# Router logits in column groups: four 384-column fp32 matmuls a chunk in place of twelve 8-column ones

## What is computed

```python
def _moe2_ref(x, modality_id, w_gate, modality_bias, w1, w2) -> np.ndarray:
    N, D = x.shape
    E = w_gate.shape[1]
    logits = x @ w_gate + modality_bias[modality_id]
    e_idx = np.argmax(logits, axis=1)
    ...
    for e in range(E):
        mask = e_idx == e
        ...
        h = np.maximum(x[mask] @ w1[e], 0.0)
        out[mask] = gate_w[mask, None] * (h @ w2[e])
```

## Time and profile before

| | |
|---|---|
| median of 3 runs | 871.68 us |
| the profiled execution's own time | 872.59 us |
| its span, first to last instruction | 870.8 us |
| TensorE (PE) busy | 857.4 us, 98% |
| VectorE (DVE) busy | 519.3 us, 60% |
| ScalarE (ACT) busy | 374.4 us, 43% |
| GpSimd (POOL) busy | 327.0 us, 38% |
| mean granted TensorE clock | 0.997 of full |

### The profile page before, as it was taken

One profiled execution on the slowest core, in us unless ns is written; L12 is line 12 of the kernel. 1 busy time (PEld: TensorE's weight loads), 2 busy tenths in 40 slices (PEclk: granted clock), 3 DMA queues, 4 the chain that ended last, 5 costly groups with the idle time before them and its releaser, 6 DMA issues.

```text
span 870.8 us, 15612 instructions
## 1 busy us (share of the span) xinstructions
PE 857.4 (98%) x5233; PEld 735.9 (84%) x5242; DVE 519.3 (60%) x1401; ACT 374.4 (43%) x945; POOL 327.0 (38%) x372
## 2 busy tenths in 40 slices
PE   8999999999999999999999999999999999999997
PEld 5677898888888888899999999988888888888885
DVE  6975555333453335449787773873877456666664
ACT  6966413545454455543221132143355335554442
POOL 3836762344333443346335332160043221222212
PEclk9999999999999999999999999999999999999999
DMA  8983212222223210242131121537265635565541
GB/s 192 286 205 97 61 48 65 74 65 78 52 52 110 62 38 26 73 157 66 45 97 61 60 74 37 193 98 254 97 195 208 248 135 187 183 223 182 186 133 45
DMA packets 77517, 103.40 MB, mean 119 GB/s; under 512 B 38973, under 2 KB 43069, under 8 KB 77312
## 3 DMA queue, kind: packets, MB, share of 16 engines
q1 hardware_dynamic: 73760, 91.16, 34.2%
q0 software_dynamic: 3680, 11.28, 3.8%
HBM read 92.98 MB, written 10.22 MB: 119 GB/s over the span
## 4 chain that ended last, share of the span: by engine, by line
PE 89%; DVE 5%; DMA 1%; issue 1%; POOL 1%; ACT 1%; SPq 1%; DVEq 0%; ACTq 0%; POOLq 0%
PE ps L1243 32%; PE ps L1282 16%; PE ps L1805 13%; PE ps L1790 12%; PE ps L1174 3%; PE ps L1203 2%; PE ps L1184 2%; PE ps L1815 2%; PE ps L1150 2%; DMA out_raw<-in_moe_w_out 1%; PE ps L1319 1%; PE ps L660 1%; DVE sm L1520 1%; DVE w_lo L2048 1%; PE ps L1312 1%
## 5 line engine op out<-in xcount | busy, mean ns | idle before, releaser
L1035 POOL TENSOR_TENSOR sm<-sm,rinv 72x288 f32<-72x288 f32 (+1 forms) x51 | 45.5, 893 | 175.3 <-DVE rinv L1531 175.2
L1067 POOL TENSOR_TENSOR out_lo<-out_raw,out_hi 128x512 fp32r<-128x512 f32 x72 | 100.6, 1397 | 5.8
L1589 DVE SCALAR_TENSOR_TENSOR h<-h,ps 128x384 f32<-128x384 f32 x72 | 39.8, 553 | 105.2 <-ACT h L1437 104.5
L1065 POOL CAST out_hi<-out_raw 128x512 fp32r<-128x512 f32 x72 | 50.1, 696 | 136.4 <-DMA out_raw<-in_moe_w_out 136.4
L1243 PE MATMUL ps<-x_hi,val_hi 128*128 128x384 f32 x288 | 101.0, 351 | 0.0
L1243 PE MATMUL ps<-x_hi,gate_hi 128*128 128x384 f32 x288 | 100.3, 348 | 0.0
L1243 PE MATMUL ps<-x_hi,gate_lo 128*128 128x384 f32 x288 | 96.9, 336 | 0.0
L1243 PE MATMUL ps<-x_hi,val_lo 128*128 128x384 f32 x288 | 96.5, 335 | 0.0
L1441 ACT ACTIVATE h_hi<-h 128x384 fp32r<-128x384 f32 x72 | 37.8, 525 | 136.5 <-DVE h L1595 136.5
L1243 PE MATMUL ps<-x_lo,val_hi 128*128 128x384 f32 x288 | 96.4, 335 | 0.0
L1243 PE MATMUL ps<-x_lo,gate_hi 128*128 128x384 f32 x288 | 93.8, 336 | 0.0
(11 more groups left out here) (278 smaller groups left out, 1944.5 us busy)
## 6 DMA issues: line engine op xcount, KB each, us to landing
w_raw<-in_moe_w SPq DMA_DIRECT2D x72, 512.0 KB, 4.8
out_raw<-in_moe_w_out SPq DMA_DIRECT2D x72, 256.0 KB, 2.7
x_rows<-y_tiles SPq DMA_DIRECT2D x18, 256.0 KB, 2.7
early_w_raw<-in_moe_w SPq DMA_DIRECT2D x8, 512.0 KB, 8.0
gate_raw<-in_moe_w_gate SPq DMA_DIRECT2D x4, 768.0 KB, 8.1
val_raw<-in_moe_w_val SPq DMA_DIRECT2D x4, 768.0 KB, 10.9
qk<-in_q SPq DMA_DIRECT2D x8, 288.0 KB
qk<-in_k SPq DMA_DIRECT2D x8, 288.0 KB
```

The lines of the kernel that those rows point to most:

```text
L1035: pool.tensor_tensor(s3, s3, rinv[0:n, i, :].unsqueeze(2).to_broadcast([n, 4, c]), ALU.mult).then_inc(s_no, 1)
L1065: pool.tensor_copy(oh[i][:, :], o_raw[i][:, :]).then_inc(s_oh, 1)
L1067: pool.tensor_tensor(ol[i][:, :], o_raw[i][:, :], oh[i][:, :].bitcast(f32), ALU.subtract).then_inc(s_ol, 1)
L1589: dve.scalar_tensor_tensor(out=hf[n % 2][:, :], in0=hf[n % 2][:, :], scalar=1.0, in1=ps[:, 0, 0:CH], op0=ALU.add, op1=ALU.mult).then_inc(s ...
```

## The change

For each of the last three chunks, the roles of the operands are swapped. `rw`, padded with zeros from 8 to 32 columns for each of the four parts of the 512 features, becomes the stationary operand, and `yT` of all three tiles (384 tokens) the moving one. The four parts `kk` of the features are not summed in PSUM: part `kk` is written to the output partitions 32kk to 32kk+31 of one bank. ScalarE copies this to `parts`, three transposes turn it back so that tokens are on partitions, and VectorE sums the four parts with one reduce and adds the bias of three tiles at once.

```diff
-Y_TILE = {(NC - 2, t): at(NC - 1, 1 + t, 0) for t in range(TT)}
-LOGITS = {k: s + 2 for k, s in Y_TILE.items()}
+Y_TILE = {(c, t): at(c + 1, 1, 1) + 2 * t for c in (NC - 3, NC - 2) for t in range(TT)}
+LOGITS = {c: Y_TILE[c, TT - 1] + 3 for c in (NC - 3, NC - 2)}
+TURN_BACK = {c: s + 2 for c, s in LOGITS.items()}
...
-for c in range(NC - 3, NC - 2):
-    free = [at(c + 1, f, 1, 1) for f in range(1, FT) if at(c + 1, f, 1, 1) not in QK_AT]
-    for t in range(TT):
-        Y_TILE[c, t], LOGITS[c, t] = free[t], free[t + 1]
...
-        rw = keep.put("rw", [P, KT, E])
+        rw = keep.put("rw", [P, KT, P // KT])
...
+            pool.memset(rw[:, :, E:P // KT], 0.0).then_inc(s_cst, 1)
...
             def turn_y(c, t):
...
+                if n >= 1:
+                    pe.wait_ge(s_yte, n)
                 for kk in range(KT):
-                    mm = pe.transpose(ps[:, y_bank(c), kk * P:(kk + 1) * P], ys[:, t, kk * P:(kk + 1) * P],
-                                      ident[:, :])
+                    mm = pe.transpose(ps[:, 6, kk * P:(kk + 1) * P], ys[:, t, kk * P:(kk + 1) * P], ident[:, :])
...
-                pe.wait_ge(s_yte, turned(c, t) + 1)
+                pe.wait_ge(s_yte, TT * i + TT)
                 for kk in range(KT):
-                    mm = pe.matmul(ps[:, logits_bank(c), 0:E], yT[:, kk, :], rw[:, kk, :],
-                                   start=(kk == 0), stop=(kk == KT - 1))
+                    mm = pe.matmul(ps[32 * kk:32 * kk + 32, 5, 0:CH], rw[:, kk, :], yT[:, kk, :], start=True, stop=True)
                 mm.then_inc(s_lg, 1)
+
+            def turn_back(c):
+                i = ROUTED.index(c)
+                pe.wait_ge(s_lc, i + 1)
+                for t in range(TT):
+                    mm = pe.transpose(ps[:, 5, t * P:(t + 1) * P], parts[:, t * P:(t + 1) * P], ident[:, :])
+                mm.then_inc(s_lt, 1)
...
+            def copy_parts(c):
+                i = ROUTED.index(c)
+                act.wait_ge(s_lg, i + 1)
+                act.activation(parts[:, :], ps[:, 5, 0:CH], ACT.Copy).then_inc(s_lc, 1)
...
+            def add_bias(c):
+                i, n = ROUTED.index(c), TT * c
+                dve.wait_ge(s_lt, i + 1)
+                dve.tensor_reduce(summed[:, :, :],
+                                  ps[:, 5, 0:CH].rearrange("p (t k e) -> p t e k", t=TT, k=KT)[:, :, 0:E, :],
+                                  axis=AX, op=ALU.add).then_inc(s_ls, 1)
+                dve.wait_ge(s_ls, i + 1)
+                dve.tensor_tensor(logit[:, n:n + TT, :], summed[:, :, :], bias_t[:, n:n + TT, :],
                                   ALU.add).then_inc(s_le, 1)
...
-            last_logits(0)
-            last_logits(1)
+            pe.wait_ge(s_ca, 2)
+            pe.wait_ge(s_cv, 1)
+            for kk in range(KT):
+                mm = pe.matmul(ps[32 * kk:32 * kk + 32, 5, 0:CH], rw[:, kk, :], yT_c[:, kk, :], start=True, stop=True)
+            mm.then_inc(s_cl, 1)
             up(0, range(KT // 2 + 1, KT))
-            last_logits(2)
+            pe.wait_ge(s_cc, 1)
+            for t in range(TT):
+                mm = pe.transpose(ps[:, 6, t * P:(t + 1) * P], parts_c[:, t * P:(t + 1) * P], ident[:, :])
+            mm.then_inc(s_cb, 1)
             turn_h(0)
             up(1, [0])
             pe.wait_ge(s_hot, 2)
...
+            act.wait_ge(s_cl, 1)
+            act.activation(parts_c[:, :], ps[:, 5, 0:CH], ACT.Copy).then_inc(s_cc, 1)
             relu(0)
...
+            dve.wait_ge(s_cb, 1)
+            link(dve, dve.tensor_reduce(summed_c[:, :, :],
+                                        ps[:, 6, 0:CH].rearrange("p (t k e) -> p t e k", t=TT, k=KT)[:, :, 0:E, :],
+                                        axis=AX, op=ALU.add))
+            link(dve, dve.tensor_tensor(logit[:, NTT - TT:NTT, :], summed_c[:, :, :], bias_t[:, NTT - TT:NTT, :],
+                                        ALU.add))
             one_hot(dve, NTT - TT, NTT)
```

More of the change, by code:

```diff
@@ L124 @@
          [("p", j) for j in TURN_AT.get(s, [])] + [("o", j) for j in PV_AT.get(s, []) if s >= EARLY]
[L125 to L126 removed]
+         + [("ss", c) for c in SS_AT.get(s, []) if c] + [("rb", c) for c in SPREAD_AT.get(s, []) if c]]
 BEFORE7 = {x: BANK7[n - 1] if n else None for n, x in enumerate(BANK7)}
[L131 to L134 removed]
 Y_AT = by_tick((k, Y_TILE[k]) for k in sorted(Y_TILE))
[L136 to L138 removed]
+LOGITS_AT = by_tick((c, s) for c, s in LOGITS.items())
+TURN_BACK_AT = by_tick((c, s) for c, s in TURN_BACK.items())
+ROUTED = (NC - 3, NC - 2)
 DOTTED = TT * (NC - 3)
@@ L275, in fused_kernel @@
         kT = [res.put(f"kT{i}", [P, WIN + S]) for i in range(2)]
-        sm = [res.put(f"sm{i}", [P, 512]) for i in range(SM - 1)] + [alias("sm_early", yT_at, [P, 512])]
+        sm = [res.put(f"sm{i}", [P, 512]) for i in range(SM - 1)] + [sm_early]
         pt = [res.put(f"pt{i}", [P, 4 * LQ]) for i in range(2)]
@@ L352, in fused_kernel @@
         dots = ra.put("dots", [P, 2, E])
+        yT = ra.put("yT", [P, KT, CH])
+        parts = ra.put("logit_parts", [P, CH])
+        summed = ra.put("logits_summed", [P, TT, E])
         re = Region(xT_at)
@@ L369, in fused_kernel @@
         rc = Region(vh_at + QB, oh_at)
-        yT_c = [rc.put(f"yT_c{i}", [P, KT, P]) for i in range(TT)]
+        yT_c = rc.put("yT_c", [P, KT, CH])
+        parts_c = rc.put("logit_parts_c", [P, CH])
+        summed_c = rc.put("logits_summed_c", [P, TT, E])
         rank8 = rc.put("rank8", [P, NTT, E])
@@ L1104, in bank_7_free @@
                     pe.wait_ge(s_nv, before[1] + 1)
-                elif before[0] == "rb":
+                else:
                     pe.wait_ge(s_rc, before[1])
[L1107 to L1110, removed]
             def residues():
@@ L1353, in front_pe @@
                     spread_roots(c)
-                for key in LOGITS_AT.get(s, []):
-                    logits(*key)
                 for key in Y_AT.get(s, []):
                     turn_y(*key)
+                for c in LOGITS_AT.get(s, []):
+                    logits(c)
+                for c in TURN_BACK_AT.get(s, []):
+                    turn_back(c)
                 if s == COUNT_1:
@@ L1473, in front_act @@
                     evac_yT(*key)
+                for c in LOGITS_AT.get(s, []):
+                    copy_parts(c)
                 if s == SPREAD[0] + 1:
@@ L1663, in front_dve @@
                     add_bias_to_dots(i)
-                for key in LOGITS_AT.get(s, []):
-                    add_bias(*key)
+                for c in TURN_BACK_AT.get(s, []):
+                    add_bias(c)
                 for val, i in SPLIT_AT.get(s - 2, []):
```

86 lines of the change are left out of this document (31 added, 55 removed).

## The result

The changed kernel takes 868.48 us (median of 7 runs, 867.06 to 872.4), the kernel before, run beside it, 871.95 us (871.12 to 873.11). The ratio is 0.9957, with a 95% interval of 0.9944 to 0.997: 0.43% faster, where 0.35% and 868.7 us were forecast. The same kernel timed twice more gave 868.4 us for 871.85 (ratio 0.9949, 0.9931 to 0.9967) and 868.67 for 871.83 (0.9953, 0.9936 to 0.9969).

A forecast was written before the change was run, and what follows sets the result against it. TensorE, busy 857.4 of 870.8 us, was taken to bound the kernel. Terms -1.20 - 1.32 - 0.77 + 0.27 = -3.0 us take the median from 871.68 to 868.7 us; range 867.9 to 871.2.

The forecast's parts named there:

- chunk 3: TensorE, routing of chunk 3: turning, logits block and turning back take 2.70 us for 3.90, that is -1.20.
- chunk 4: TensorE, routing of chunk 4: turning, logits block and turning back take 2.70 us for 4.02, that is -1.32.
- chunk 5's logits: TensorE, chunk 5: block of 1.02 us replaces two tiles' logits of 1.79, -0.77; turning back free in the relu wait.
- the reduce, paid in full: VectorE's chain to `hot_b`, start of experts' part: added reduce costs +0.27 us (0.21 to 0.33), since TensorE already waits.
- All four groups at once: Logits block on TensorE: four column groups overlap fully, two steps, 0.64 us of streams; chance 0.68 with no new wait.
- serial rival: Logits block: passes run one after another, block 2.95 us, sum +2.8 us, 874.5 us; chance 0.08.
- two-at-once rival: Logits block: only two groups run at once, block 1.66 us, sum -1.1 us, 870.6 us; chance 0.12.
- The fixed price: Logits block on TensorE: going to narrow column groups and back costs 0.37 us, the same for both lengths read.
- What costs nothing: ScalarE's copies, new waits of the turns, GpSimd's memset, SyncE: covered by other work, slack 1 us and more, 0 us.
- new-wait rival: Routing chunks: late `h_lo` or an uncovered copy takes 0.5 to 1.5 us of the gain, 869.2 to 870.2; chance 0.12.
- layout theory: Follow-up forecast: buffer places shorten untouched stretches, median 0.3 to 0.9 us under the kernel before, 3.0 over the changed.
- its rival: Follow-up forecast: buffer places do nothing, same time within 0.3 us, 3.5 us over the changed kernel; no chance given.

The follow-up runs named there:

- one wide group: Changed kernel with router weights taken 128 columns wide, all four matmuls accumulating in one place, no column groups: 874.49 us for 871.74, ratio 1.0028.
- two groups: Changed kernel with router weights padded to 64 columns, four matmuls on two column groups, reduce summing two parts: 872.41 us for 871.74, ratio 1.0001.
- doubled block: Changed kernel with the four logits matmuls of each block issued a second time, same result, without leaving the groups: 869.65 us for 871.74, ratio 0.9969.
- layout kernel: Kernel before with only its buffers' SBUF places as in the changed one, router's work untouched: 871.93 us for 871.83, ratio 1.0002.

## Why the prediction was right, step by step

| step of the prediction | forecast, us | from the stretches |
|---|---|---|
| chunk 3 | -1.20 | 80.46 to 79.24: -1.22 |
| chunk 4 | -1.32 | 103.16 to 101.79: -1.37 (-1.12 and -1.30 in the other two profiles) |
| chunk 5's logits | -0.77 | 7.34 to 6.56: -0.78 |
| the reduce, paid in full | +0.27 | 2.74 to 3.03: +0.29 |
| sum | -3.0 | -3.1 |
| not in the prediction | | the untouched stretches: -0.8 (-0.4 in the second profile of the changed kernel) |

**All four groups at once.** This was the step on which the sign hung, and it held. From one wide group to two groups to four the block goes 2.57, 1.64, 0.98 us. The doubled block gives the fixed price by itself, 2 x 0.98 - 1.63 = 0.33 us; take it off the narrow ones, and 2.57, 1.31 and 0.65 remain: the streams overlap fully at each size. The rows of single passes show the same, four starts together and four more 0.35 us later. The serial rival wanted 2.95 us and the two-at-once rival 1.66; both fall. The Trainium skill (TensorE: Matmul & The Clock Gate, Part 3, "The mechanism") lets LDWEIGHTS overlap matmuls in flight only when the row group differs; here all four groups use the same 128 rows, their second weights are loaded at 447.47 while the first four matmuls run from 447.44 to 447.97, and so this trace disagrees, and the measurement decides. Its 2.38 times for three groups (same part, "Measured speedup vs the span model") would have made the streams 0.81 us, an estimate; for these four they take 0.65, a quarter of 2.57.

**The fixed price.** 0.37 us was taken over from two groups of 64 to four of 32, with 0.01 added for later starts. Measured, it is 0.98 - 0.64 = 0.34, so the block was put 0.04 us too high in chunk 3 and, with 1.00 us measured, 0.02 in chunk 5. The starts show where it lies: the block begins 0.09 us later than an ordinary step, the second four come 0.03 later than a stream takes, the next product 0.12 after their end, and the product behind it is another 0.11 late. That it is paid for a visit and not for a pass was read from two lengths only; the doubled block shows it directly.

**The reduce on the chain** was the only cost forecast, and the row that it was read from, the weight load for `hot_b`, went from 0.48 to 0.78 us, where 0.75 was forecast. The prediction took the 0.48 for the time that TensorE stands, and that was too much: by the starts it was 0.22 us late, and 2.74 - 2.59 = 0.15 us is what came back when the wait was gone. Any wait above zero makes an added link count in full, so the sum did not suffer. "Paid in full" was right of this order of VectorE's work, not of the reduce as such: with the reduce ahead of the rows' low part nothing is paid. The prediction looked at what the reduce delays, and not at whether the engine stands idle earlier with the operand ready.

**What costs nothing** cost nothing. There is no wait for `yT` or the parts, and the wait for `h_relu` is the half microsecond in which the third tile's logits were free. The new-wait rival falls: the 0.4 us for `h` are in the second profile of the kernel before as well. ScalarE's copy in chunk 5 runs from 599.51 to 600.00, under the matmuls that reach to 600.89.

**What was off.** The prediction calls 1.1 us the longest wait of PE. Its list has a longer one, 1.5 us for `warm` at the program's start, which the change does not touch. The upper end of its range, 871.2 us, lies 0.6 over the two-groups case, where 0.4 is named as the spread. PE's busy time fell by 5.1 us and not by about 4. And the total fell by 3.5, 3.5 and 3.2 us in the three comparisons of medians, a little more than the 3.0. The profile has that surplus where the change does nothing: 238.03 - 237.52 = 0.51 us over the expert steps and 0.30 over the three chunks before the routing. With only the layout changed these are there too (0.45 and 0.31), less the 0.23 us by which its two stretches with routing are longer. This is a term that the prediction did not have, and one that only the profiles show. Against the layout kernel, run on the same chip, the router's work alone is 871.93 - 868.67 = 3.3 us by the medians, between the 3.0 of the layout theory and the 3.5 of its rival; resampling the two sets of runs leaves anything from 2 to 5 us, so it decides nothing.

## What to carry to other kernels

A matmul with few output columns can be dealt out over column groups by its contraction tiles: four fp32 matmuls of 384 columns cost here what one costs, 0.64 us, and 0.34 us for the visit. So it pays only with enough work a visit, and the parts have to be turned, summed and covered by other work, which is where a link on a waiting chain can give a part back. When a link is added to such a chain, look first for idle time of that engine after the operand is there: moving it ahead of a waiting operation made it free. And where a change moves buffers, cost it against a kernel with only the buffers moved; a few tenths of a microsecond in the profile's stretches came with that alone.

## What had not been expected of the hardware

The runs of one kernel spread by 3 to 6 us, and most of it goes with the mean granted clock. One slope fitted to all timed runs, some 150 of eight kernels, is 0.58 us (give or take 0.05) for each 0.001 of clock, and takes up four fifths of the variance within the kernels. At full clock that puts the kernel before at 870.7 us and the changed one at 866.7 to 867.1 in its three sets. In the profiles the clock goes at one place, behind a stretch in which TensorE is kept waiting. Busy time by engine from 40 to 55 us (the three figures at the end are the granted clock, the DMA share and GB/s), first the kernel before:

```profile
40.00:55.00 15.00, 13.48 (x127) 9.06 (x127) 12.40 (x71) 11.15 (x49) 6.00 (x7) 0.89 0.83 175
```

and the same kernel in its second profile:

```profile
40.00:55.00 15.00, 14.08 (x146) 9.45 (x145) 13.70 (x73) 12.56 (x57) 6.66 (x7) 1.00 0.81 178
```

The second execution has 4.10 us in the same window and stays at 1.00. So the same kernel has the fall in one execution and not in the other, and the first stretch, from the sums of squares of chunk 0 to those of chunk 1, is 87.81 us in the one and 86.46 in the other. It lies far ahead of the router's work, and this spread is what makes a difference of half a microsecond hard to time.
